# A three-part transformer kernel on one core: weight combinations moved to GpSimd, the first block of the large stage in halves, transposes moved into a wait

## The reference, cut to what matters

```python
def _moe_ref(x, phi, w1, w2):            # 3072 tokens x 512, 8 experts, 4 slots each
    logits = x @ phi                     # phi: 512 x 32
    d = softmax of logits over tokens
    slot_input = (d.T @ x).reshape(8, 4, 512)
    for e in range(8):
        h = np.maximum(slot_input[e] @ w1[e], 0.0)    # w1[e]: 512 x 1024
        slot_out[e] = h @ w2[e]                       # w2[e]: 1024 x 512
    c = softmax of logits over the 32 slots
    return c @ slot_out.reshape(32, 512)

def _moe2_ref(x, w_in, w_out):           # the large stage
    h = x @ w_in                         # 512 x 2048
    r = np.maximum(h, 0.0)
    return (r * r) @ w_out               # 2048 x 512

def reference(q, k, v, ...):
    x = local attention with a few global keys (4 x 8 heads, 768 tokens)
    return _moe2_ref(_moe_ref(x))
```

## Time and profile before

| | |
|---|---|
| median of three runs | 506.81 us |
| the profiled execution, as timed | 506.44 us |
| its span in the trace | 504.6 us |
| TensorE busy | 480.8 us, 95% of the span |
| TensorE loading weights | 398.9 us |
| VectorE busy | 363.3 us, 72% |
| ScalarE busy | 346.3 us, 69% |
| GpSimd busy | 94.8 us, 19% |
| the chain that ended last | TensorE 80%, ScalarE 9%, VectorE 5%, issue 3% |

### The profile page before, as it was taken

The page is one execution under the profiler, slowest core; times in us unless marked ns, Lnnn a source line. Parts: engine busy times, 40 slices in busy tenths (PEclk is TensorE's granted clock), DMA queues, the critical chain, the costliest instruction groups (busy, mean ns, idle before and its releaser), DMA issues.

```text
span 504.6 us, 12853 instructions
## 1 busy us (share of the span) xinstructions
PE 480.8 (95%) x4608; PEld 398.9 (79%) x4608; DVE 363.3 (72%) x1026; ACT 346.3 (69%) x761; POOL 94.8 (19%) x223
## 2 busy tenths in 40 slices
PE   2999999999999998799899999999999999999996
PEld 1667677777667643337789999999999999999996
DVE  6687877787787661318989978777687777768782
ACT  2788897897898610016999887776777776777740
POOL 1555454545445403300000000000000000000000
PEclk9999999999999999989999999999999999999999
DMA  7699889884565799993001011010110101001011
GB/s 284 255 348 361 353 307 336 320 311 166 193 202 189 279 350 410 420 400 129 1 0 44 2 43 42 0 42 0 42 42 0 42 0 42 21 21 42 0 43 42
DMA packets 17979, 77.24 MB, mean 153 GB/s; under 512 B 2320, under 2 KB 2320, under 8 KB 14352
## 3 DMA queue, kind: packets, MB, share of 16 engines
q1 hardware_dynamic: 14720, 60.95, 32.8%
q10 hardware_dynamic: 3216, 15.73, 8.1%
HBM read 70.39 MB, written 6.29 MB: 152 GB/s over the span
## 4 chain that ended last, share of the span: by engine, by line
PE 80%; ACT 9%; DVE 5%; issue 3%; POOL 1%; DMA 1%; DVEq 0%; ACTq 0%; POOLq 0%
PE bank L1629 14%; PE bank L1628 14%; PE bank L1630 14%; ACT probs L1027 5%; PE bank L1288 5%; PE bank L1600 4%; PE bank L1276 4%; PE bank L1303 4%; PE bank L1557 3%; PE bank L1530 3%; PE bank L1308 2%; PE bank L1349 2%; PE bank L1328 2%; POOL probs L463 1%; DVE probs L553 1%
## 5 line engine op out<-in xcount | busy, mean ns | idle before, releaser
L1027 ACT ACTIVATE probs<-probs,nmax 128x232 f32<-128x232 f32 (+1 forms) x192 | 88.6, 463 | 31.0 <-DVE nmax L553 30.1
L463 POOL TENSOR_SCALAR probs<-probs,rden 128x232 f32<-128x232 f32 (+1 forms) x192 | 82.9, 452 | 88.6 <-DVE rden L562 88.6
L1628 PE MATMUL bank<-t_hi,s_hi 128*128 128x256 f32 x352 | 98.7, 280 | 0.0
L1629 PE MATMUL bank<-t_lo,s_hi 128*128 128x256 f32 x352 | 98.6, 280 | 0.0
L1630 PE MATMUL bank<-t_hi,s_lo 128*128 128x256 f32 x352 | 98.5, 280 | 0.0
L1150 ACT ACTIVATE g_s<-bank 128x1024 f32<-128x1024 f32 x48 | 48.9, 1022 | 30.2 <-PE bank L1600 30.2
L1179 ACT ACTIVATE s_hi<-s 128x512 fp32r<-128x512 f32 x88 | 55.0, 627 | 18.4 <-DVE s L954 14.6
L1628 PEld LDWEIGHTS bank<-t_hi,s_hi 128*128 128x128 f32 x352 | 66.5, 189 | 0.0
L1629 PEld LDWEIGHTS bank<-t_lo,s_hi 128*128 128x128 f32 x352 | 66.4, 189 | 0.0
L1630 PEld LDWEIGHTS bank<-t_hi,s_lo 128*128 128x128 f32 x352 | 66.4, 189 | 0.0
L877 DVE TENSOR_TENSOR s_lo<-s,s_hi 128x512 fp32r<-128x512 f32 x88 | 56.9, 687 | 6.8 <-DVE s L954 3.5
(11 more groups left out here) (194 smaller groups left out, 1025.8 us busy)
## 6 DMA issues: line engine op xcount, KB each, us to landing
qkv_s<-qkv_dram SPq DMA_DIRECT2D x15, 1028.0 KB, 7.3
qkv_s<-qkv_dram SPq DMA_DIRECT2D x16, 704.0 KB, 5.4
w_s<-w_dram ACTq DMA_DIRECT2D x5, 2048.0 KB, 12.0
w_s<-w_dram SPq DMA_DIRECT2D x13, 512.0 KB, 8.6
out_dram<-o_stage SPq DMA_DIRECT2D x24, 256.0 KB, 2.0
wo_raw<-w_out_dram SPq DMA_DIRECT2D x4, 1024.0 KB, 14.5
w_a<-w_dram SPq DMA_DIRECT2D x3, 1024.0 KB, 11.7
w_a<-w_dram SPq DMA_DIRECT2D x5, 512.0 KB, 6.4
```

Of the source, the lines that this page charges most:

```text
L463: last = pool.tensor_scalar(probs[:, v % 2, m, a, 0:w], probs[:, v % 2, m, a, 0:w], rden[:, v % 2, m, a:a + 1], 1.0, ALU.mult, ALU.mult)
L1027: act.activation(probs[:, v % 2, m, a, 0:w], probs[:, v % 2, m, a, 0:w], ACT.Exp, bias=nmax[:, v % 2, m, a:a + 1], scale=-1.0, accum_out=d ...
L1628: pe.matmul(OUT[n], hi, W_HI[n](at_f), start=(c == 0 and f == 0 and n in (0, 2, 4, 5)), stop=False, skip_group_check=True)
L1629: pe.matmul(OUT[n], hi, W_LO[n](at_f), start=False, stop=False, skip_group_check=True)
```

## The change

Six edits, all between the second expert group and the end of block 0:

- TensorE: `parts(2)` and `parts(3)` both stand ahead of `l2_1`, with four and three idle products behind them; the four idle products ahead of row block 7 become one.
- VectorE: `spread` is written after the experts' last copy, and lies elsewhere in memory.
- TensorE: `hidden(0,0,0)` runs after the first half of the spreading instead of after both. The two idle products ahead of `hidden(0,1,0)` go, the seven behind it become one.
- ScalarE: the first of block 0's four pieces (128x1024) is worked in two halves of 128x512: relu, square, high part for the first 128 tokens, then the same for the second.
- VectorE keeps two of the eight weight combinations (t0, t2 of half 0). GpSimd makes the other six.
- VectorE: the copy of `m3` moves ahead of the second `wo_low`.

```diff
+            for c in range(2):                                  # GpSimd
+                fs = slice(GF * c, GF * c + GF)
+                if c == 1:
+                    pool.wait_ge(wo_in[1], 16)
+                    pool.wait_ge(mid_pe, pe_at["m3"])
+                    pool.tensor_tensor(t_32[0][:, fs, :], blk(1, 1), blk(1, 0), ALU.subtract).then_inc(t_made, 1)
+                    pool.wait_ge(wo_in[3], 16)
+                    pool.tensor_tensor(t_32[2][:, fs, :], blk(3, 1), blk(1, 1), ALU.subtract).then_inc(t_made, 1)
+                else:
+                    pool.wait_ge(wo_in[2], 16)
+                pool.wait_ge(t_made, 4 * c + MADE[2])
+                pool.tensor_tensor(t_32[1][:, fs, :], blk(2 + c, 1), t_32[0][:, fs, :], ALU.subtract).then_inc(t_made, 1)
+                pool.wait_ge(t_made, 4 * c + MADE[1])
+                pool.tensor_tensor(t_32[3][:, fs, :], t_32[1][:, fs, :], blk(2 + c, 0), ALU.subtract).then_inc(t_made, 1)
...
             wo_low(0, 0)                                        # VectorE
             copy_mix(1)
-            combine(0, (1,))
             plain_low(0, 0)
             plain_low_second(0, 0)
-            combine(0, (3,))
+            copy_mix(3)
             wo_low(0, 1)
-            copy_mix(3)
             plain_low(0, 1)
             plain_low_second(0, 1)
-            combine(1, (0, 2))
             wo_low(1, 0)
-            combine(1, (1,))
             plain_low(1, 0)
             plain_low_second(1, 0)
-            combine(1, (3,))
             wo_low(1, 1)
...
+            def plain_high_halves(to):                          # ScalarE
+                act.wait_ge(h_ready, 1)
+                at_t = to * P
+                half = g_s[0][:, 0, :, at_t:at_t + P]
+                from_h = banks[:, 0:1024].rearrange("p (f n) -> p f n", f=GF)[:, :, at_t:at_t + P]
+                if to == 0:
+                    act.activation(half, from_h, ACT.Relu).then_inc(half_made, 1)
+                    act.wait_ge(half_made, 1)
+                    act.activation(half, half, ACT.Square).then_inc(half_made, 1)
+                    act.wait_ge(half_made, 2)
+                    act.activation(a_hi[:, 0, :, :], half, ACT.Copy).then_inc(hi_done, 1)
+                else:
+                    act.activation(half, from_h, ACT.Relu).then_inc(relu_done, 1)
+                    act.wait_ge(relu_done, 1)
+                    act.activation(half, half, ACT.Square).then_inc(squared, 1)
+                    act.wait_ge(squared, 1)
+                    act.activation(s_hi[:, 0, :, :], half, ACT.Copy).then_inc(hi_done, 1)
...
+                if g == 1:                                      # TensorE, ahead of l2_1
+                    parts(2)
+                    idle_products(4, 7)
+                    parts(3)
+                    idle_products(3, 7)
                 for f in range(FEC):
-                    if g == 1 and f in (0, FEC // 2):
-                        parts(3 if f else 2)
...
-                            idle_products(4, 3)
+                            idle_products(1, 3)
```

More of the change, by code:

```diff
@@ L117, in build @@
         w2_s0 = at(REG_A, "w2_s0", [P, FEC, D])
+        spread = at(REG_A, "spread", [P, 4, 6, SLOTS], F32R, start=w2_at)
         w2_a = at(REG_A, "w2_a", [P, 2 * FEC, D], start=0)
@@ L327, in before, with blk @@
             return (b, s - lag) if s >= lag else (b - 1, s - lag + STEPS)
+        def blk(n, half):
+            return wo_raw[:, 4 * n:4 * n + 4, half * HD:(half + 1) * HD]
         block = ctx.enter_context(nc.Block())
@@ L809, in _, with combine_rows @@
                                      bank[7][:, :].rearrange("p (c j r) -> p c j r", c=DC, j=4)[:, :, :, 0:SPE]), f"so_t_{g}")
-            def blk(n, half):
-                return wo_raw[:, 4 * n:4 * n + 4, half * HD:(half + 1) * HD]
-            def combine(c, which):
+            for r, times in ((0, 0.0), (2, 1.0), (4, 0.0)):
+                own(dve.tensor_scalar(spread[:, :, r:r + 2, :], ident[:, :].rearrange("p (n s) -> p n s", n=4).unsqueeze(2)
+                                      .broadcast_to([P, 4, 2, SLOTS]), times, None, ALU.mult), S2)
+            def combine_rows(c, j):
                 fs = slice(GF * c, GF * c + GF)
[L816 to L827, removed]
-                        dve.tensor_tensor(t_32[3][:, fs, :], t_32[1][:, fs, :], blk(2 + c, 0), ALU.subtract).then_inc(t_made, 1)
+                dve.wait_ge(wo_in[(c, None, 2 + c)[j]], 16)
+                if j == 0:
+                    dve.tensor_tensor(t_32[0][:, fs, :], blk(c, 1), blk(c, 0), ALU.subtract).then_inc(t_made, 1)
+                else:
+                    dve.tensor_tensor(t_32[2][:, fs, :], blk(2 + c, 1), blk(c, 1), ALU.subtract).then_inc(t_made, 1)
             def wo_low(c, u):
@@ L1580, in _, with spread_mix @@
                 mark(last, f"mix_{h}")
-            for h in range(2):
+            def spread_mix(h):
                 pe.wait_ge(mid_act, act_at[f"mix_gh_{h}"])
@@ L1656, in _ @@
             for u in range(2):
[L1657 to L1658 removed]
+                spread_mix(u)
+                if u == 0:
+                    pe.wait_ge(mix_act, 1)
+                    hidden(0, 0, 0, True)
+            pe.wait_ge(mix_act, 2)
+            hidden(0, 0, 1, True)
             pe.wait_ge(mix_dve, 1)
[L1660 removed]
             hidden(0, 1, 0, False)
[L1662 removed]
+            idle_products(1, 6)
             plain(0)
```

18 lines of the change are left out of this document (6 added, 12 removed).

## The result

The changed kernel takes 509.98 us (median of six runs, 508.77 to 510.78) against 506.75 (six runs, 506.24 to 508.01): a ratio of 1.006, 95% interval 1.0042 to 1.0078. It is slower by about 3 us. The forecast of 505.1 was wrong in sign, and the time lies outside the range of 504.1 to 507.6. The profiled execution took 509.28 with a span of 507.5, 2.9 more than before.

The account below looks back on a forecast made before the run. ScalarE's chain was taken to bound 234 to 251 us. Gains 1.6 + 0.8 - 0.45 = 1.95, less 0.2 for GpSimd, give 1.75: profiled 506.44 becomes 504.7, plus 0.37 for the median 505.1 us; range 504.1 to 507.6.

Parts of the forecast that it names:

- Bound and view: From 234 to 251 us ScalarE's gapless chain is the bound and sets TensorE's product of 251.02.
- Part 1: Last expert layer: transposes and idle products fill earlier idleness, so row block 7 starts at 223.0, not 224.6; gain 1.6 us.
- Rival (e): Last part of the expert weights lands later, so the last expert layer gives 0.6, not 1.6: 506.1 us; chance 0.07.
- Part 2: First hidden product: starts 1.4 us after the spreading's start instead of 2.22; gain 0.8 us.
- Part 3: ScalarE's first piece in halves: relu to next `wo_high` takes 3.68 us instead of 3.21; cost 0.45 us.
- The sum of the three: Parts 1 to 3 together: 1.6 + 0.8 - 0.45 = 1.95 us earlier at `wo_high` and the product of 251.02.
- Part 4: Six combinations on GpSimd at 2.45 us each: just in time; 0.2 us of loss put into the sum.
- GpSimd ran at about half its rate, VectorE at full: Contention read from attention's scalings: 0.16 us lost in an overlap of at most 0.30, all by GpSimd.
- due time: When GpSimd's combinations are needed: two at 237.1, four at 242.1, all six at 251.1 us.
- (a): GpSimd's combinations come too late and become the bound, slower than before: 508.1, or 510.8 with both bad; chance 0.13.
- (c): Clock falls in TensorE's longer wait at 247 to 249 us, price 1.3 us, giving 506.4; chance 0.08.
- (d): ScalarE's chain is not the bound, TensorE's lead from the earlier plain block counts: 2.8 us, 504.0; chance 0.05.

Follow-up runs that it names:

- experiment 5: Kernel before with only both batches' transposes and the idple products moved ahead of the last expert layer: 505.47 us, ratio 0.9974.
- experiment 8: Changed kernel with all combinations on VectorE, four idle products in the wait for ScalarE, first `t_hi` after the last plain piece: 504.16 us, ratio 0.9954.
- experiment 1: Changed kernel with all eight weight combinations on VectorE, other edits kept: 505.92 us, ratio 0.9987 to the kernel before.
- experiment 10: Changed kernel with GpSimd's six two-input subtractions replaced by one-input scalings of the same size: 505.44 us, ratio 0.9972 to the kernel before.
- experiment 4: Changed kernel with each of GpSimd's six combinations written as four instructions of 128x256: 509.88 us, ratio 1.0073 to the kernel before.
- experiment 9: Changed kernel with all combinations on VectorE, first piece whole, first `t_hi` behind last plain piece, three idle products in ScalarE wait: 504.09 us, ratio 0.9944.
- experiment 2: Kernel before with only six of eight combinations moved to GpSimd and VectorE's order that goes with it: 511.68 us, ratio 1.0104.

## Why the prediction was wrong, point by point

**Bound and view: right.** ScalarE's chain set the product of 251.02. Where it is moved alone (experiment 5) the product and the end move with it; where one `t_hi` is taken out of it (experiment 8) the product comes 0.9 us sooner in the trace, the time 0.6 us sooner with overlapping intervals.

**Part 1, forecast 1.6 us: right.** 1.66 in the trace of experiment 5. The weights land where they land: row block 7 started between 222.65 and 224.01 in the profiles, and in the changed kernel at 223.38 it gained 1.3 only. Rival (e) lives in this spread. No window near 215 is below 1.00, as foreseen.

**Part 2, forecast +0.8: right.** From the spreading to the first `hidden` it is 231.22 - 229.79 = 1.43 us, forecast 1.4. At ScalarE's relu 0.7 of the 0.8 are left (232.00 - 229.79 = 2.21, before 233.92 - 231.03 = 2.89).

**Part 3, forecast -0.45: right,** 0.43. The sum of the three at the product was 1.78 where 1.95 was forecast (experiment 1).

**Part 4: the step that failed** is "GpSimd ran at about half its rate, VectorE at full". Neither half of it holds in general. The 0.16 us of rows 11 and 12 were read as half a rate over 0.3 us of overlap, but standing still fits them as well: VectorE's instruction ends at 15.70, and 0.456 - 0.13 more, the same 0.13 as above, is 16.03, where GpSimd's first scaling ends (15.41 + 0.615 = 16.03). An overlap that short can't tell the two; experiment 10 can, and there GpSimd stands still for the whole of VectorE's instruction. "VectorE at full" holds nearly for an instruction of GpSimd with one input. I carried it over to instructions with two inputs, which no row showed. With two inputs VectorE is shut out for GpSimd's whole instruction, and I had priced VectorE's delay at nothing; it measured 11.7 us over six instructions, and came to TensorE as waits of 2.24 and 1.70 us. For `hidden(0,1,0)` the prediction named only ScalarE's relu and put it at 234.0; it began at 235.61, released by VectorE's copy of `m1`. The sizes were fair: GpSimd's own time is 2.25 us (I took 2.45), and the six were over at 250.1, before the 251.1 at which I had put their due time. (The 10.6 us of VectorE's work in that sum are 10.4 by its own terms, which changes nothing.) The due times were the wrong question. VectorE's own parts, `copy_mix(1)` at 234.9 and `a_lo` at 247.8, became late from 16 us before that point on.

The section "Who interferes with whom" of the page SBUF — State Buffer in the Trainium skill has this rule, and I had read only the shorter sentence of the GPSIMD Engine Reference: the pair of ports that VectorE and GpSimd share is held for a whole instruction, and whichever comes second stands still (the Trainium skill says this last of VectorE's two-port modes, under its general rule that the pair is an exclusive lock); a VectorE instruction with two SBUF inputs takes it against any GpSimd instruction that reads SBUF. The trace agrees for GpSimd's two-input instructions, by 0.68 us that became 2.26 to 2.92. For one-input ones it agrees where GpSimd comes second (4.91 for 2.77), and doesn't where VectorE does: its 0.68 became 1.13 at most (experiment 10) beside a GpSimd instruction of 3.51 us. The estimate of 2.25 us from the GPSIMD Engine Reference of the Trainium skill, section 3.1, was right, by the steps from 232.8 on.

**Rivals.** (a) had the sign, and the measured 509.98 lies between its 508.1 and 510.8, but that is luck: its mechanism (GpSimd too late, VectorE waiting for it) wasn't the one, as VectorE never waits for GpSimd in the changed kernel's profile; only experiment 4 made it so. (c) came true once parts 1 to 3 stood alone: I had priced it at 1.3 us, and it cost 1.6 in the execution that shows it. In the changed kernel the clock fell elsewhere, in a wait that I hadn't foreseen. (d) is out: in experiment 1 the plain block began 2.55 us earlier than before (235.04 against 237.59), the product behind it only 1.78, and the rest is in TensorE's wait, 2.09 us where it was 1.36.

## What to carry to other kernels

Before work moves to GpSimd beside a busy VectorE, count the SBUF inputs on both sides. Two and two excluded each other for whole instructions here, so the price is one GpSimd instruction for each instruction of VectorE that somebody waits for, and it is paid far ahead of the due time of what was moved. And when a chain is shortened, look at how long the engine that waits for it now idles: an idle stretch may cost as much clock as the shortening gave (1.6 of 1.8 us in experiment 1), and idle products can hold the clock, but where they end after the wait they are a delay themselves (0.5 us in experiment 9).

## What the runs showed of the hardware that I had not expected

- The exclusion between GpSimd and VectorE with two SBUF inputs on each side (2.28 to 4.20 us, 0.68 to 2.92), and that ScalarE (`wo_high` 1.89 us beside it, 1.91 before) and VectorE's copies out of PSUM (0.68) feel nothing of it.
- That it is lopsided with one input on GpSimd: VectorE loses 0.0 to 0.6 us, and GpSimd all that is left of VectorE's instruction (4.91 for 2.77).
- TensorE's granted clock fell to 0.50 after waits of 2.24 us (the change), 2.09 (experiment 1), 1.78 and 2.51 (experiment 4); it stayed at 1.00 through waits of 1.36 and 1.30, of 1.70 in the changed kernel, 1.86 in experiment 10 and 2.51 in experiment 2. So the length of one wait doesn't decide it between 1.7 and 2.6 us; what does wasn't found.
- In 33 runs of the kernel before, the eight with a mean clock of 1.000 took 504.63 to 505.99 us, and the other 25 took 506.17 to 508.7. A part of what looks like noise thus goes with the clock; whether the clock makes it, or a later landing makes both, isn't shown. In which wait it fell isn't known for runs without a trace; the profiled one shows it at 214 us.
